# Weight order, a second tile taken straight from PSUM, and two low parts moved to VectorE in a convolution + two-layer MLP kernel

## What is computed

```python
w = softmax(weight)                       # 8 heads x 7 taps
x1[b,s,:] = sum_k w[head,k] * x_pad[b,s+k,:]      # causal convolution, 7 taps
h = x1 @ w_in
P = a0 + a1*h + a2*h**2 + a3*h**3
Q = 1 + |b0|*|h| + |b1|*h**2
g = P / (Q + 1e-6)
x2 = g @ w_out                            # layer 1
r = maximum(x2 @ w2_in, 0)
out = (s*r*r + b2) @ w2_out               # layer 2
```

## Time and profile before

| | before |
|---|---|
| median of 3 runs | 1266.43 us (1266.32 to 1266.73) |
| profiled execution, its own time | 1267.56 us |
| its span, first to last instruction | 1265.7 us |
| PE busy / weight loads | 1250.9 us (99%) / 1078.0 us (85%) |
| DVE busy | 1119.9 us (88%) |
| ACT busy | 1073.1 us (85%) |
| POOL busy | 331.4 us (26%) |
| chain that ended last | PE 90%, DVE 6%, the rest 4% |

### The profile page before, as it was taken

One profiled execution on the slowest core, in us unless ns is written; L12 is line 12 of the kernel. 1 busy time (PEld: TensorE's weight loads), 2 busy tenths in 40 slices (PEclk: granted clock), 3 DMA queues, 4 the chain that ended last, 5 costly groups with the idle time before them and its releaser, 6 DMA issues.

```text
span 1265.7 us, 16270 instructions
## 1 busy us (share of the span) xinstructions
PE 1250.9 (99%) x6018; PEld 1078.0 (85%) x6018; DVE 1119.9 (88%) x1031; ACT 1073.1 (85%) x1091; POOL 331.4 (26%) x153
## 2 busy tenths in 40 slices
PE   7999999999999999999999999999999999999999
PEld 5767888888888888888888888888888888888888
DVE  7997999998999989998999989999899998888740
ACT  6898888988989888888888889898898888888853
POOL 3443222322222222223223222222232232222210
PEclk8999999999999999999999999999999999999999
DMA  7100000010000100000000100001000000000000
GB/s 223 61 10 17 1 13 1 1 39 0 12 0 12 25 0 12 0 12 25 11 1 0 38 0 12 0 0 38 0 12 0 12 0 1 13 1 13 1 13 13
DMA packets 14748, 20.39 MB, mean 16 GB/s; under 512 B 1792, under 2 KB 9984, under 8 KB 14592
## 3 DMA queue, kind: packets, MB, share of 16 engines
q1 hardware_dynamic: 14576, 20.01, 5.4%
q10 hardware_dynamic: 144, 0.01, 0.0%
HBM read 13.72 MB, written 6.29 MB: 16 GB/s over the span
## 4 chain that ended last, share of the span: by engine, by line
PE 90%; DVE 6%; issue 1%; DMA 1%; ACT 1%; SPq 1%; POOL 0%; DVEq 0%; ACTq 0%
PE o L454 26%; PE h L436 5%; PE h L437 5%; PE h L441 4%; PE h L446 4%; PE h L447 4%; PE o L426 4%; PE h L405 4%; PE h L409 4%; PE o_tail L427 4%; PE h L407 4%; PE h L406 4%; PE h L408 4%; PE o_tail L420 4%; PE o L419 4%; PE o L418 4%
## 5 line engine op out<-in xcount | busy, mean ns | idle before, releaser
L394 POOL TENSOR_TENSOR gl<-work,gh 128x1024 fp32r<-128x1024 f32 x128 | 309.5, 2418 | 830.0 <-ACT gh L677 822.6
L454 PE MATMUL o<-v,work 128*128 128x192 f32 x2048 | 353.3, 326 | 0.9 <-issue 0.9
L454 PEld LDWEIGHTS o<-v,work 128*128 128x128 f32 x2048 | 339.1, 190 | 11.1 <-issue 1.3
L667 ACT ACTIVATE work<-h,coef 128x1024 f32<-128x1024 f32 x128 | 154.3, 1205 | 135.1 <-PE h L409 134.3
L881 DVE SCALAR_TENSOR_TENSOR work<-work,coef,h 128x1024 f32<-128x1024 f32 x128 | 163.8, 1280 | 74.8 <-ACT work L668 72.4
L911 DVE SCALAR_TENSOR_TENSOR work<-work,coef 128x1024 f32<-128x1024 f32 x128 | 164.5, 1285 | 4.5
L887 DVE SCALAR_TENSOR_TENSOR work<-work,coef,h 128x1024 f32<-128x1024 f32 x128 | 164.0, 1281 | 4.5
L905 DVE SCALAR_TENSOR_TENSOR work<-work,coef 128x1024 f32<-128x1024 f32 x128 | 164.1, 1282 | 0.0
L907 DVE SCALAR_TENSOR_TENSOR work<-work 128x1024 f32<-128x1024 f32 x128 | 159.0, 1242 | 4.4
L884 DVE TENSOR_TENSOR work<-work,h 128x1024 f32<-128x1024 f32 x128 | 155.4, 1214 | 0.0
L710 ACT ACTIVATE work<-h 128x1024 f32<-128x1024 f32 x128 | 130.3, 1018 | 23.9 <-PE h L447 23.8
(11 more groups left out here) (101 smaller groups left out, 2015.3 us busy)
## 6 DMA issues: line engine op xcount, KB each, us to landing
out_dram<-y_out SPq DMA_DIRECT2D x32, 192.0 KB, 2.0
xt<-in_x_main_dram SPq DMA_DIRECT2D x7, 518.0 KB, 5.0
xt_tail<-in_x_tail_dram SPq DMA_DIRECT2D x8, 259.0 KB, 5.3
work<-in_moe_w_out_dram SPq DMA_DIRECT2D x2, 768.0 KB, 8.6
v<-in_moe_w_out_dram SPq DMA_DIRECT2D x1, 1536.0 KB, 6.2
raw_w_tail_late<-in_moe_w_in_dram SPq DMA_DIRECT2D x4, 256.0 KB, 7.1
work<-in_moe_w_in_dram SPq DMA_DIRECT2D x2, 512.0 KB, 5.7
xt<-in_x_main_dram SPq DMA_DIRECT2D x2, 259.0 KB, 7.6
```

Source lines behind the costliest of these rows:

```text
L394: nc.gpsimd.tensor_tensor(gl[:, j % 2, :], r_buf[j % 2], gh[:, j % 2, :].bitcast(F32), ALU.subtract).then_inc(gl_ready, 1)
L454: return pe.matmul(o2[:, c // 2, c % 2, 0:D], g, v2[:, f, :], start=(f == 0 and c % 2 == 0), stop=(f == FT - 1), skip_group_check=True)
L667: nc.scalar.activation(t_of_n, h_flat, ACT.Identity, bias=a2, scale=a3).then_inc(t_ready, 1)
```

## The change

Six edits; nothing of the arithmetic changes.

1. SP issues the two halves of v1 ahead of piece 1 of w1. ACT's casts of piece 1 move from before the v1 casts to between `first_steps(0)` and `first_steps(1)`. The counts that wait on `w_hi_ready` follow.
2. x1 of the second tile no longer goes through SBUF: ACT casts `conv_bank[1]` directly to `x1_hi[1]` at unit 2 (it copied it to `conv` at unit 3), and DVE makes `x1_lo[1]` from PSUM at unit 3. Its 64 tail rows are cast by ACT and subtracted by POOL at the very start. DVE's four instructions of `split_conv(0, 1)` at unit 5 go. `conv_copied` counts one less.
3. The bias row is made by ACT at unit 5 and not by DVE at unit 4.
4. `late_exponential` is true from unit 9 (it was from unit 11), so the Exp of units 9 and 10 stands one unit later in ACT's order.
5. ACT's copy of `conv_tail` at the third unit of the second tile moves from the end of that unit to before its Abs.
6. `gl` of the last two units (126, 127) is made by DVE, that of 126 between L905 and L907 of unit 127; POOL leaves them out.

```diff
--- before.py
+++ after.py
@@ -62,7 +62,8 @@
                7: (("pair_b", (3, 4, 5, 6)),), 8: (("tail", (0, 1, 2)),), 9: (("tail", (3, 4, 5, 6)),)}
 
     SPLIT_A, SPLIT_A_FIRST = (1, 5), (1, 6)
-    SPLIT_B, SPLIT_B_OF_FIRST = (1, 7), (0, 5)
+    SPLIT_B = (1, 7)
+    FIRST_SECOND_SPLIT = 3
 
     def at(i, usual, start):
         return start if isinstance(i, int) and i == 0 else usual
@@ -195,6 +196,7 @@
         x2_lo_ready, x2_sum_ready = sem("x2_lo_ready"), sem("x2_sum_ready")
         x2_tail_hi_ready, x2_tail_lo_ready = sem("x2_tail_hi_ready"), sem("x2_tail_lo_ready")
         y_ready_out = sem("y_ready_out")
+        x1_tail_second = sem("x1_tail_second")
 
 
 
@@ -234,7 +236,11 @@
 
         def late_exponential(n):
 
-            return not isinstance(n, int) or n > SKEW
+            return not isinstance(n, int) or n >= SKEW - 1
+
+        def by_vector(n):
+
+            return isinstance(n, int) and n >= NU - 2
 
         def is_end(n):
             return isinstance(n, int) and n == NU
@@ -289,10 +295,10 @@
             sp.dma_start(coef[:, 4:6], b.partition_broadcast(P)).then_inc(coef_loaded, 16)
             sp.dma_start(coef[:, 6:7], s.partition_broadcast(P)).then_inc(coef_loaded, 16)
             sp.dma_start(coef[:, 7:8], b2.partition_broadcast(P)).then_inc(coef_loaded, 16)
-            load_w1(1)
             for half in range(2):
                 f = V1_HALF[half]
                 sp.dma_start(raw_v1[:, f], w_out1[:, f]).then_inc(v1_loaded[half], 16)
+            load_w1(1)
             sp.dma_start(xt[:, 1, :], x_main[:, 1, 0:HALO + TOK]).then_inc(x0_second_loaded, 16)
             load_w1(2)
 
@@ -356,7 +362,13 @@
             low_of_w1(slice(2 * P, TOK), 1)
 
             pool.wait_ge(w_ready, 1)
-            low_of_w1(PIECES[1], 3)
+
+            pool.wait_ge(x1_tail_second, 1)
+            pool.wait_ge(w_lo_ready, 4)
+            nc.gpsimd.tensor_tensor(x1_tail[1][0:TAIL, :], conv_tail[TAIL:P, :], x1_tail[1][TAIL:P, :].bitcast(F32),
+                                    ALU.subtract).then_inc(x1_tail_second, 1)
+            pool.wait_ge(x1_tail_second, 2)
+            low_of_w1(PIECES[1], 7)
 
             pool.wait_ge(w_ready, 2)
             pool.wait_ge(t3_done, 1)
@@ -389,7 +401,7 @@
                     if j == X2_STEP and tile(t - 1):
 
                         pool.wait_ge(x2_tail_lo_ready, counted(t))
-                    if unit(n - 2):
+                    if unit(n - 2) and not by_vector(n - 2):
                         pool.wait_ge(gh_ready, counted(n - 1))
                         nc.gpsimd.tensor_tensor(gl[:, j % 2, :], r_buf[j % 2], gh[:, j % 2, :].bitcast(F32),
                                                 ALU.subtract).then_inc(gl_ready, 1)
@@ -484,7 +496,7 @@
                         conv_taps(1, xt[:, 1, :], taps, 0, TAPS - 1)
                     if group == "pair_a":
                         if starts:
-                            pe.wait_ge(conv_copied, 1)
+                            pe.wait_ge(x1_lo_ready, 4)
                             pe.wait_ge(x_loaded, 32)
                         conv_taps(1, xt[:, 0, :], taps, 0, TAPS - 1)
                     if group == "pair_b":
@@ -494,7 +506,7 @@
                     if group == "tail":
                         pe.wait_ge(diag_ready, TAPS + taps[-1] + 1)
                         if starts:
-                            pe.wait_ge(conv_copied, 2)
+                            pe.wait_ge(conv_copied, 1)
                         conv_taps(1, xt_tail[:, :], taps, 0, TAPS - 1, tail_diag)
 
 
@@ -531,7 +543,7 @@
                     pe.wait_ge(x1_lo_ready, counted((t + 1) * 2))
                 if first(t) and j in (1, 2, 4, 6):
 
-                    high, low = {1: (2, 4), 2: (4, 6), 4: (10, 9), 6: (10, 10)}[j]
+                    high, low = {1: (2, 4), 2: (8, 6), 4: (10, 9), 6: (10, 10)}[j]
                     pe.wait_ge(w_hi_ready, high)
                     pe.wait_ge(w_lo_ready, low)
 
@@ -557,7 +569,7 @@
 
                         tk = t + (j - SKEW - OUT2_LAG) // UNITS
                         pe.wait_ge(y_ready_out, counted(tk * 2))
-                        pe.wait_ge(conv_copied, 4)
+                        pe.wait_ge(conv_copied, 3)
                         pe.wait_ge(v2_loaded, 16)
                     pe.wait_ge(g2_ready, counted(m - OUT2_LAG + 1))
                     second_product_2(k, (j - OUT2_LAG) % 2)
@@ -650,8 +662,9 @@
             high_of_w1_tail(0)
             for k in range(4, TAPS):
                 diagonal(k, 0)
-            high_of_w1_main(1)
-            high_of_w1_tail(1)
+
+            act.wait_ge(tail_step, TAPS)
+            nc.scalar.copy(x1_tail[1][TAIL:P, :], conv_tail[TAIL:P, :]).then_inc(x1_tail_second, 1)
             for half in range(2):
                 f = V1_HALF[half]
                 act.wait_ge(v1_loaded[half], 16)
@@ -692,15 +705,24 @@
                         first_steps(n, h1_flat, t_buf, w_abs)
                     if first(t) and j == 0:
 
+                        high_of_w1_main(1)
+                        high_of_w1_tail(1)
                         first_steps(1, h2_flat, num_buf[1], q_buf[1])
                         high_of_w1_main(2)
                         high_of_w1_tail(2)
+                    if first(t) and j == 5:
+                        act.wait_ge(colsum_ready, 1)
+                        nc.scalar.activation(bias_row[:, :], o2[:, 0, 0, 0:D], ACT.Identity,
+                                             scale=b2_col).then_inc(bias_row_ready, 1)
                     if is_end(n):
                         exponential(n - 1, 1 - buf)
                     if unit(n - 2) and not cast_early(n - 2):
                         high_of_g(n - 2, buf)
                     if unit(n - 1) and late_exponential(n - 1) and not is_end(n):
                         exponential(n - 1, 1 - buf)
+                    if second(t) and j == 2:
+                        act.wait_ge(conv_summed, 5)
+                        copy_of_conv(conv_tail[:, :], 1)
                     if unit(n):
                         act.wait_ge(z_done, counted(n + 1))
                         nc.scalar.activation(q_buf[buf], q_buf[buf], ACT.Abs).then_inc(q_ready, 1)
@@ -723,9 +745,10 @@
                         high_of_g(n - 1, 1 - buf)
                     if unit(n) and not late_exponential(n):
                         exponential(n, buf)
-                    if first(t) and j == 3:
+                    if first(t) and j == 2:
+
                         act.wait_ge(conv_summed, 2)
-                        copy_of_conv(conv[:, 1, :], 1)
+                        nc.scalar.copy(x1_hi[1][:, :], conv_bank[1]).then_inc(x1_hi_ready, 2)
                     if first(t) and j == 6:
                         act.wait_ge(conv_summed, 3)
                         act.wait_ge(x1_lo_ready, 2)
@@ -734,9 +757,6 @@
                         act.wait_ge(conv_summed, 4)
                         act.wait_ge(x1_lo_ready, 4)
                         copy_of_conv(conv[:, 1, :], 0)
-                    if second(t) and j == 2:
-                        act.wait_ge(conv_summed, 5)
-                        copy_of_conv(conv_tail[:, :], 1)
                     if isinstance(n, int) and n in W2_HIGH_AT:
                         rows, half = W2_HIGH_AT[n]
                         if rows == "main":
@@ -781,10 +801,8 @@
 
                 high, low = tail_rows[batch], tail_rows[1 - batch]
                 done = pair * 2 + batch
-                if isinstance(done, int) and done == 1:
-                    dve.wait_ge(conv_copied, 1)
-                elif isinstance(pair, int) and pair == 1:
-                    dve.wait_ge(conv_copied, 4)
+                if isinstance(pair, int) and pair == 1:
+                    dve.wait_ge(conv_copied, 3)
                     dve.wait_ge(tail_step, counted(tail_steps(pair)))
                 else:
                     dve.wait_ge(main_step, counted(main_steps(pair)))
@@ -859,8 +877,8 @@
             dve.wait_ge(w_lo_ready, 4)
             for half in range(2):
                 f = V1_HALF[half]
-                low_of_weight(v1_lo[:, f, :], raw_v1[:, f, 0:P], v1_hi[:, f, :], 5 + 2 * half)
-                low_of_weight(v1_tail[:, f, 1, :], raw_v1[:, f, P:D], v1_tail[:, f, 0, :], 6 + 2 * half)
+                low_of_weight(v1_lo[:, f, :], raw_v1[:, f, 0:P], v1_hi[:, f, :], 3 + 2 * half)
+                low_of_weight(v1_tail[:, f, 1, :], raw_v1[:, f, P:D], v1_tail[:, f, 0, :], 4 + 2 * half)
             dve.wait_ge(coef_loaded, 64)
             dve.wait_ge(coef_ready, 2)
 
@@ -896,13 +914,22 @@
                                 y_out[:, 2 * half:2 * half + 2, :], o2[:, half, :, 0:D], s_col,
                                 bias_row[:, :].unsqueeze(1).broadcast_to([P, 2, D]),
                                 ALU.mult, ALU.add).then_inc(y_ready_out, 1)
-                    if first(t) and (parity, j) == SPLIT_B_OF_FIRST:
-                        split_conv(i, 1)
```

(15 more changed lines are left out.)

## The result

| | before | after |
|---|---|---|
| median | 1266.62 us (1266.32 to 1267.27, 6 runs) | 1261.6 us (1260.64 to 1262.06, 6 runs) |
| ratio after / before | | 0.9958, 95% interval 0.9946 to 0.9971 |
| profiled execution, its own time | 1267.56 us | 1262.06 us |
| its span | 1265.7 us | 1260.3 us |

The median of before has moved from 1266.43 to 1266.62, since three more executions of that kernel are in it. The two profiled executions differ by 5.5 us.

A forecast was written before the change was run, and what follows sets the result against it. PE was taken to bound the middle, leaving gains only before about 105 us and at layer 1's end: 3.2 (first x2) + 1.0 (copy) + 1.8 (end) = 6.0 us, from 1266.43 to 1260.4, range 1258.8 to 1263.3.

The forecast's parts named there:

- the x2 step: ACT's first x2 cast, at 95.19: PE's last sum sets it at 91.95, gaining 3.2 us.
- Order of the weights: Start: v1 is issued and lands 1.6 us earlier, between 0 and 1.9, moving `first_steps(0)` with it.
- Casts moved, first L905: Unit 0: casts behind `first_steps(0)` cost ACT 1.04 us, so DVE's first L905 gains 0.8 instead of 1.6.
- PE's second product: Start on PE: DVE's L887 and POOL's low part end together, so it starts near 23.5, gaining 1.6 us.
- The clock: PE's 1.2 GHz stretch, 25 to 30 us: may vanish; g's low part caps PE's gain at 1.6 to 2.3, 1.95 taken.
- Second tile and bias row: DVE, units 4 and 5: the split taken off gains 1.63 us, the bias row some 0.35.
- Copy of conv_tail: Before L454 at 105.52: moved ahead, the copy hides in ACT's wait for DVE, gaining 1.0 us.
- The end: End of layer 1: gl(126), L907 and L911, and gl(127) meet PE's 1211.0, 1214.15 and 1215.5, gaining 1.8 us.
- A: Rival at the start: v1 lands no earlier, gain 4.1 us, time 1262.3 us; chance 0.12.
- B: Rival at the start: PE has slack up to 94 us, ACT alone sets x2; gain 6.6, time 1259.8; chance 0.10.
- C: Rival at the end: L907's 3.41 us isn't due to POOL and stays; gain 4.2, time 1262.2; chance 0.08.
- D: Rival, first ten units: POOL's work reaches into L905 or L907, DVE waits 17.4 us; time 1277.8; chance 0.04.

The follow-up runs named there:

- old_order: Changed kernel with the weights' transfers and the casts of w1 piece 1 back in their old places: 1261.80 us.
- warm_casts_old: `warm_casts` with the old order of the weights' transfers and of the casts of w1 piece 1: 1262.62 us.
- dve_work_back: Changed kernel with the split at unit 5 and the bias row back on DVE: 1262.91 us, ratio 0.9970.
- copy_as_before: Changed kernel with ACT's copy of conv_tail back at the end of its unit: 1261.37 us.
- warm_casts: Changed kernel with the additions of both `warm` and `casts_later`: 1261.98 us.
- hold_w1: Changed kernel, but SP waits for both halves of v1 before issuing w1 piece 1, the second tile's x and w1 piece 2: 1264.77 us, ratio 0.9985.
- end_only: Kernel before with only the low parts of units 126 and 127 moved to DVE: 1265.13 us, ratio 0.9989.
- exp_as_before: Changed kernel with the Exp of unit 9 ahead of x2's cast again: 1262.12 us.
- casts_later: Changed kernel with ACT's two casts of w1 piece 2 behind Exp(0) and the first cast of g ahead of Ln(1): 1262.33 us.
- warm: Changed kernel with five unread 128-column matmuls on PE behind the first convolution part, so PE isn't idle before its second product: 1261.31 us.
- the pair of longer kernels: Four unread matmuls added on PE in unit 3, to the kernel before (1266.83 us) and to the changed kernel (1262.54 us).

## Why the prediction was right, point by point

- *What bounds the kernel.* Right: all of the gain lies ahead of L454 and at the end of layer 1, and from L454 to the end nothing else moved by more than 0.2 us. The gain of 5.0 us by the medians lies at the lower edge of the 5 to 7 that the prediction called its forecast; the x2 step gave 2.48 us for 3.2.
- *Order of the weights.* The term was mis-sized. It was put at 1.6 us, taken over from SP's issue; the two profiles show 0.69, and the medians with and without it differ by 0.2 (`old_order`) and 0.6 (`warm_casts_old`), less than their runs spread, so that anything from 0 to about 1 us is possible and 1.6 isn't. The second v1 cast starts at 17.18, 16.58, 16.00, 16.29 and 16.63 in the five profiles with the old order, and between 14.12 and 16.48 in the eight with the new one that hold nothing back: 1.1 us earlier in the mean, but `first_steps(0)` gains only 0.7 in the mean (18.24 to 17.52). Where v1 was early, `first_steps(0)` waited for PE's first product instead: 17.07, 17.17, 17.34 and 17.00 in `dve_work_back`, `copy_as_before`, `warm_casts` and `hold_w1`.
- *The execution it was read from.* The profile of before has the latest `first_steps(0)` of its order, and lies 1.13 us above the first median and 0.94 above the new one. What follows `first_steps(0)` is the same to 0.1 us in the three profiles with the old start (1248.68; 1248.59; and 1246.85 + 1.83 for `end_only`), although the lower clock lasted over 6 us in two of them and 3.4 in the third. So a middling execution should have it at about 1266.62 - 1248.68 = 17.9 instead of 18.88; that is worked out, not measured, since only profiled executions show it. The prediction mentioned the 1.13 us and didn't ask where they lay. Part of what the edit was to gain was a delay of that one execution.
- *Casts moved, first L905.* The mechanism was right, its place was off with the term before: 28.89 for 27.87, of which the weights' term is 0.9. DVE was put at 0.8 us earlier here and was 0.2 later.
- *PE's second product.* Right about the tie of two conditions; POOL decided it. 24.44 for 23.5, and nearly all of that is the weights' 0.9.
- *The clock.* Left open, between a low stretch as before and none. It was low for 3.4 us in the profile, and not at all in those of `exp_as_before` and `casts_later`, although PE was idle there for 2.64 and 2.81 us ahead of its second product; the length of the idle stretch alone doesn't decide it. The cap by the first low part of g was right and its place was wrong: POOL starts it at 33.95 for 34.06, 0.1 us earlier and not 1.1, and PE takes it at 36.41, right behind its end at 36.35. So PE had gained 1.3 us at this point and could not have gained more; at its last sum it is 1.19 for the 1.95 of the prediction. `warm` shows PE waiting there when the clock stays up.
- *Second tile and bias row.* 2.0 us on DVE, right; `dve_work_back` shows 1.25 of it in the time, the rest hidden behind PE's route.
- *First x2.* Right that PE's last sum would set it. 92.71 for 91.95.
- *Copy of conv_tail.* 1.03 for 1.0, but credited to the wrong edit alone: moving the Exp is enough by itself, and so is moving the copy.
- *The end.* 1.83 for 1.8, and each of the three dates held: all parts came in time and PE has no gap there.
- *Rivals.* A describes the median better than expected: its 4.1 and the forecast's 6.0 lie to both sides of the measured 5.0. B fell with the pair of longer kernels: the share of weight loads said nothing on PE's slack here, the distances between starts did. C fell with `end_only`. D didn't happen in the changed kernel, where L927 and L934 never last over 1.29; its mechanism did in `casts_later`. The Trainium skill (GPSIMD Engine Reference, Specifications) names this contention; the runs agree, with 2.20 and 2.17 us for 1.23 and 1.28.

What stays open: why the second v1 cast starts up to 2.4 us apart from one execution of the new order to the next, and by how much exactly edit 1 is worth, somewhere from 0 to about 1 us.

## What to carry to other kernels

Ask of a profiled execution that lies above its median where it is late, before costing an edit at that very place. Where two routes meet at one instruction, write down both arrival times: a gain counts up to the other route, and the test is to lengthen one route by a known piece of work before and after. Before moving GpSimd work with SBUF operands, look at which VectorE instructions it will lie beside.

## What the runs showed of the hardware

A `scalar_tensor_tensor` on DVE with two SBUF inputs and a subtraction on POOL hold each other up, and in more than one way. At the end of the kernel before, DVE alone paid: 3.41 us instead of 1.22, POOL kept its 2.40:

```profile
1208.83 2.40 POOL L394 TENSOR_TENSOR gl<-work,gh 128x1024 fp32r<-128x1024 f32 x1 [5.33 <-ACT gh L677]
```

In `casts_later` both paid, 2.20 and 2.17 on DVE, 2.3 each on POOL for what takes 1.27. Which of the two pays goes with which started first. POOL's instruction above started 0.07 us ahead of L907 and kept its length, and L907 took about the rest of it longer. In `casts_later` DVE's L930, with two SBUF inputs too, started 0.05 us ahead of POOL's first (27.33 and 27.38) and kept its 1.28, and POOL's first took 2.38. DVE's instructions that read h from PSUM aren't held up: L902 lasts 1.21 to 1.22 in all 128 units of the changed kernel. Here is one on VectorE beside one on GpSimd in the changed kernel, both at their usual length:

```profile
21.73 1.21 DVE L902 TENSOR_TENSOR work<-work,h 128x1024 f32<-128x1024 f32 x1
```

```profile
21.83 1.27 POOL L352 TENSOR_TENSOR w_lo<-v,w_hi 128x512 fp32r<-128x512 f32 x1
```

The table's own surprise is how well one number tells a kernel apart: from `first_steps(0)` to L454, kernels with the same order after that point agree within 0.2 us (86.50 to 86.65, 83.63 to 83.82, 84.54 to 84.76), while their own times spread over 1.1 to 1.3.
